# A gated linear-attention kernel: carries over pairs of runs, run ends copied by ScalarE, and the scale's clamp folded into one product

## The reference

```python
mag = np.sqrt(a_re * a_re + a_im * a_im)
scale = np.minimum(mag, 0.999) / (mag + 1e-06)
a_re_n, a_im_n = (a_re * scale, a_im * scale)
for t in range(S):
    ar, ai = (a_re_n[:, :, t, :, None], a_im_n[:, :, t, :, None])
    new_re = ar * S_re - ai * S_im
    new_im = ar * S_im + ai * S_re
    kv = np.einsum('bhd,bhe->bhde', k[:, :, t], v[:, :, t])
    S_re, S_im = (new_re + kv, new_im)
    y[:, :, t] = np.einsum('bhd,bhde->bhe', q[:, :, t], S_re)
...
h = x @ w_in
g = np.maximum(h, 0.0) + np.log1p(np.exp(-np.abs(h)))
x = g @ w_out
...
a = x @ w1
b = x @ w2
h = a * b @ w3
out = h @ w_out2
```

## Time and profile before

| | |
|---|---|
| median of 3 runs | 986.51 us (985.63 to 987.29) |
| profiled execution, its own time | 987.42 us |
| its span in the trace | 985.6 us |
| PE busy | 900.9 us (91%) |
| DVE busy | 608.7 us (62%) |
| ACT busy | 426.5 us (43%) |

### The profile page before, as it was taken

How to read it: one execution, slowest core, us unless ns; L and a number is a source line. 1 busy time by engine, 2 the same in 40 slices (tenths; PEclk the granted TensorE clock), 3 DMA queues, 4 the chain that set the end, 5 groups by cost and what they waited for, 6 DMA issues and landing times.

```text
span 985.6 us, 14230 instructions
## 1 busy us (share of the span) xinstructions
PE 900.9 (91%) x5298; PEld 802.6 (81%) x5298; DVE 608.7 (62%) x982; ACT 426.5 (43%) x612; POOL 70.1 (7%) x56
## 2 busy tenths in 40 slices
PE   0973838999999999999999999999999999999998
PEld 0543738989989989989889999999888888888887
DVE  5978878989988998898999833355221212121211
ACT  4142263575574584674665654588112120202011
POOL 0000000000000000000000000000222222222221
PEclk9995668999999999999999999999999999999999
DMA  9666066174263382480570460320101010101000
GB/s 336 242 192 192 20 178 149 27 213 123 99 167 97 107 191 67 130 207 26 151 199 13 115 143 13 131 105 26 56 0 65 1 65 1 64 0 64 0 33 32
DMA packets 97877, 99.49 MB, mean 101 GB/s; under 512 B 6928, under 2 KB 88848, under 8 KB 97808
## 3 DMA queue, kind: packets, MB, share of 16 engines
q1 hardware_dynamic: 97808, 98.59, 34.8%
HBM read 63.96 MB, written 29.88 MB: 95 GB/s over the span
## 4 chain that ended last, share of the span: by engine, by line
PE 62%; DVE 22%; ACT 6%; DVEq 5%; issue 3%; DMA 1%; ACTq 1%; SPq 0%
PE ps L1318 7%; PE ps L1320 7%; PE ps L1319 7%; PE ps_p L1318 7%; PE ps_p L1320 7%; PE ps_p L1319 7%; PE ps_ay L1354 3%; DVE sp L1196 2%; DVE an L1022 2%; PE ps_ay L1320 2%; PE ps_ay L1319 2%; PE ps_ay L1318 2%; PE ps_k L1320 2%; PE ps_k L1319 2%; PE ps_k L1318 2%
## 5 line engine op out<-in xcount | busy, mean ns | idle before, releaser
L1318 PE MATMUL ps<-g_h,wo_h 128*128 128x384 f32 x384 | 133.3, 347 | 2.0 <-DVE g_l L1203 2.0
L649 POOL TENSOR_TENSOR abl<-ab,abh 128x512 fp32r<-128x512 f32 x48 | 69.2, 1442 | 908.6 <-DVE abh L1301 908.6
L1320 PE MATMUL ps<-g_h,wo_l 128*128 128x384 f32 x384 | 129.6, 338 | 0.0
L1319 PE MATMUL ps<-g_l,wo_h 128*128 128x384 f32 x384 | 129.3, 337 | 0.0
L1318 PE MATMUL ps_p<-x1h,win_h 128*128 128x384 f32 x336 | 116.8, 348 | 6.1 <-DVE sp L1196 6.1
L1320 PE MATMUL ps_p<-x1h,win_l 128*128 128x384 f32 x336 | 112.7, 335 | 0.0
L1319 PE MATMUL ps_p<-x1l,win_h 128*128 128x384 f32 x336 | 112.5, 335 | 0.0
L1354 PE MATMUL ps_ay<-stq,stk 96*128 96x128 f32 x384 | 56.9, 296 | 39.6 <-DVE am L1145 15.4
L1354 PEld LDWEIGHTS ps_ay<-stq,stk 96*128 96x128 f32 x384 | 53.8, 208 | 41.8 <-issue 26.0
L1292 DVE TENSOR_TENSOR ab<-ps_ay,bc 128x512 f32<-128x512 f32 x24 | 16.6, 692 | 114.6 <-ACT bc L918 114.6
L765 ACT ACTIVATE g_h<-sp 128x768 fp32r<-128x768 f32 (+1 forms) x71 | 55.4, 780 | 65.9 <-DVE sp L1196 65.5
(11 more groups left out here) (160 smaller groups left out, 1993.6 us busy)
## 6 DMA issues: line engine op xcount, KB each, us to landing
qk_scr<-tt SPq DMA_DIRECT2D x16, 576.0 KB, 5.1
stq<-qk_scr SPq DMA_DIRECT2D x48, 192.0 KB, 4.8
qk_scr<-pp SPq DMA_DIRECT2D x16, 576.0 KB, 4.0
stk<-qk_scr SPq DMA_DIRECT2D x48, 192.0 KB, 4.5
an<-in_a_re SPq DMA_DIRECT2D x8, 576.0 KB, 3.9
an<-in_a_im SPq DMA_DIRECT2D x8, 576.0 KB, 5.3
qk<-in_q SPq DMA_DIRECT2D x8, 576.0 KB, 7.6
qk<-in_k SPq DMA_DIRECT2D x8, 576.0 KB, 8.9
```

Source lines behind the costliest of these rows:

```text
L649: tensor_tensor(abl[:, m % AR, :], ab[:, m % 2, :], abh[:, m % AR, :].bitcast(F32), ALU.subtract).then_inc(ab_lo, 1)
L1318: mm(o, wh, xh, start=start, stop=False)
L1319: mm(o, wh, xl, start=False, stop=False)
L1320: return mm(o, wl, xh, start=False, stop=stop)
```

## The change

- The carries are computed over pairs of runs: `carry in` multiplies each odd place by the even one before it (72 products of each part), `carry` 1, 2, 4, 8, 16 double over the 24 pair products (w = 24 - s), and `carry out` multiplies the even places by the pair products before them (w = 23). Before there were six doublings over 48 (w = 48 - s).
- The three copies of the run ends move from VectorE to ScalarE (`prep_ends`). VectorE signals `runs_made` behind run 7 and waits for `ends_out` in `ends`.
- `scale start` is gone: the clamp is the first operation of `scale`, as min(r, 1/0.999), and r - 1e6 comes from ScalarE (`prep_root_less`, a copy of 1152 elements with a bias) with the two semaphores `prep_root_made` and `prep_less`.
- Order. In the tables, `ends` and `carry 1` no longer stand ahead of `mask_scores` in step 2: behind it come `ends` and `carry in`, behind the sum `carry` 1 and 2, and 4, 8, 16 and `carry out` in step 3 ahead of its mask. The list `between` in the head changes likewise. In the head, `raw_low(1)` moves between `newton` and `scale`, and `raw_low(3)` from the middle of prep(0)'s carries to behind prep(1)'s `m2`. SP's `load_piece(6)` moves behind `stack_k(0, ...)`. On ScalarE, `prep_root_less(n+3)` stands in step 6 behind `g_high(n, 7)`, ahead of `softplus(n+1, 0)`, and `prep_ends(n+2)` in step 2 behind `k_by_tokens`, between `Abs` and `Exp`.

```diff
-            for i in range(3, 7):
+            for i in range(3, 6):
                 load_piece(i)
...
             for c in range(NCH):
                 stack_k(0, c)
+            load_piece(6)
             load_qk(1)
...
+            def prep_ends(m):
...
+                eng.wait_ge(runs_made, m + 1)
+                for c in range(2):
+                    act(carries[:, c, :, 1:1 + most].rearrange("p g (k r) -> p g k r", r=CR),
+                        ends[:, c, :, 0:NCH - 1, RUN - 1, :], ACT.Copy)
+                act(carries[:, :, :, 1 + most:NR], ends[:, :, :, NCH - 1, RUN - 1, 0:CR - 1], ACT.Copy).then_inc(ends_out, 1)
+
+            def prep_root_less(m):
+                eng.wait_ge(prep_root_made, m + 1)
+                act(te[:, 0, :], te[:, 1, :], ACT.Copy, bias=-1e6).then_inc(prep_less, 1)
...
             raw_high(1)
+            prep_root_less(0)
             raw_high(2)
+            prep_ends(0)
             raw_high(3)
             prep_psquares(0)
             prep_inverse(0)
             prep_squares(1)
             prep_log(1)
             prep_rsqrt(1)
+            prep_root_less(1)
...
                 if i == 1:
+                    prep_ends(1)
                     raw_high(7)
...
             g_high(0, 0, False)
+            prep_root_less(2)
...
                             if att:
                                 k_by_tokens(n + 1, j)
+                            if has_prep and j == 2:
+                                prep_ends(n + 2)
...
                         softplus(n, j + 1, split)
                         g_high(n, j + 1, split)
+                        if nxt_prep:
+                            prep_root_less(n + 3)
...
-            def prep_scale_start(m):
-                ve.tensor_scalar(tr[:, :], te[:, 1, :], 0.999, 1.0, ALU.mult, ALU.min)
-                eng.drain()
...
             def prep_scale(m):
-                ve.scalar_tensor_tensor(out=tr[:, :], in0=te[:, 1, :], scalar=-1e6, in1=tr[:, :],
-                                        op0=ALU.add, op1=ALU.mult)
+                eng.wait_ge(prep_less, m + 1)
+                ve.scalar_tensor_tensor(out=tr[:, :], in0=te[:, 1, :], scalar=1.0 / 0.999, in1=te[:, 0, :],
+                                        op0=ALU.min, op1=ALU.mult)
...
+            def prep_carry_in():
+                t = gp[:, :, :].rearrange("p c (a l) -> p c a l", l=2)
+                n = GC * CR // 2
...
             def prep_carry(s_):
 
-                w = NR - s_
+                w = NPAIR - s_
...
-            before_mask = {0: steps("a", 1), 1: steps("run", 3, 4), 2: steps("run", 7) + ["ends"] + steps("carry", 1),
-                           3: steps("carry", 8, 16, 32), 4: by[3:] + ["p"], 5: []}
-            after_mask = {0: steps("run", 1), 1: steps("run", 5), 2: steps("carry", 2), 3: by[:2], 4: [("q", 0)], 5: ["inverse"]}
-            after_sum = {0: steps("run", 2), 1: steps("run", 6), 2: steps("carry", 4), 3: by[2:3], 4: [("q", 1), "p2"], 5: ["keys"]}
+            before_mask = {0: steps("a", 1), 1: steps("run", 3, 4), 2: steps("run", 7),
+                           3: steps("carry", 4, 8, 16) + ["carry out"], 4: by[3:] + ["p"], 5: []}
+            after_mask = {0: steps("run", 1), 1: steps("run", 5), 2: ["ends", "carry in"], 3: by[:2], 4: [("q", 0)], 5: ["inverse"]}
+            after_sum = {0: steps("run", 2), 1: steps("run", 6), 2: steps("carry", 1, 2), 3: by[2:3], 4: [("q", 1), "p2"], 5: ["keys"]}
...
-            prep(0, True, ["newton", "scale start", "scale"] + steps("a", 0, 1) + steps("run", 1, 2))
+            prep(0, True, ["newton"])
             raw_low(1)
+            prep(0, True, ["scale"] + steps("a", 0, 1) + steps("run", 1, 2))
             prep(0, True, steps("run", 3, 4, 5, 6, 7))
             raw_low(2)
-            prep(0, True, ["ends"] + steps("carry", 1, 2, 4))
+            prep(0, True, ["ends", "carry in"] + steps("carry", 1, 2, 4, 8, 16) + ["carry out"] + by + ["p", ("q", 0), ("q", 1), "p2", "inverse", "keys", "keys end"], first=True)
+            prep(1, False, ["m2"])
             raw_low(3)
-            prep(0, True, steps("carry", 8, 16, 32) + by + ["p", ("q", 0), ("q", 1), "p2", "inverse", "keys", "keys end"], first=True)
-            prep(1, False, ["m2", "newton", "scale start", "scale"] + steps("a", 0, 1))
+            prep(1, False, ["newton", "scale"] + steps("a", 0, 1))
...
-            between = [steps("run", 5), steps("run", 6), steps("run", 7), ["ends"] + steps("carry", 1),
-                       steps("carry", 2, 4), steps("carry", 8, 16), steps("carry", 32) + by[:1], by[1:3], by[3:], [], ["p"], []]
+            between = [steps("run", 5), steps("run", 6), steps("run", 7), [],
+                       ["ends", "carry in"], steps("carry", 1, 2), steps("carry", 4, 8, 16) + ["carry out"] + by[:1],
+                       by[1:3], by[3:], [], ["p"], []]
...
-            prep(2, True, ["newton", "scale start", "scale"] + steps("a", 0))
+            prep(2, True, ["newton"])
             g_low(0, 0, False)
+            prep(2, True, ["scale"] + steps("a", 0))
```

More of the change, by code:

```diff
@@ L31 @@
 CR = CT // RUN
+NPAIR = NR // 2
 GC = G * NCH
@@ L178, in build @@
         prep_rs = sem("prep_rs")
+        prep_root_made = sem("prep_root_made")
+        prep_less = sem("prep_less")
         prep_p = sem("prep_p")
@@ L183, in build @@
         end_ev = sem("end_ev")
+        runs_made = sem("runs_made")
+        ends_out = sem("ends_out")
         te_free = sem("te_free")
@@ L698, in prep_rsqrt @@
                 prep_root_square(m, first)
+            def prep_ends(m):
+                carries = gp[:, :, :].rearrange("p c (g r) -> p c g r", g=G)
+                ends = an[:, :, :].rearrange("p c (g k i r) -> p c g k i r", g=G, i=RUN, r=CR)
+                most = (NCH - 1) * CR
+                eng.wait_ge(runs_made, m + 1)
[6 more added lines that the diff above has]
+                act(te[:, 0, :], te[:, 1, :], ACT.Copy, bias=-1e6).then_inc(prep_less, 1)
             def prep_psquare(m, i):
@@ L941, in _ @@
             carries = gp[:, :, :].rearrange("p c (g r) -> p c g r", g=G)
+            pairs = gp[:, :, :].rearrange("p c (g m l) -> p c g m l", g=G, l=2)[:, :, :, :, 1]
             def cmul(out_r, out_i, a, br, bi, m1, m2):
@@ L948, in cmul @@
                 ve.tensor_tensor(out_r, m1[:, 0], m2[:, 1], ALU.subtract)
-                ve.tensor_tensor(out_i, m1[:, 1], m2[:, 0], ALU.add)
+                last = ve.tensor_tensor(out_i, m1[:, 1], m2[:, 0], ALU.add)
                 eng.drain()
+                return last
             def prep_m2_(m):
@@ L964, in prep_newton @@
                 ve.scalar_tensor_tensor(out=te[:, 1, :], in0=tr[:, :], scalar=1.5, in1=te[:, 1, :],
-                                        op0=ALU.add, op1=ALU.mult)
-                eng.drain()
-            def prep_scale_start(m):
-                ve.tensor_scalar(tr[:, :], te[:, 1, :], 0.999, 1.0, ALU.mult, ALU.min)
+                                        op0=ALU.add, op1=ALU.mult).then_inc(prep_root_made, 1)
                 eng.drain()
             def prep_scale(m):
-                ve.scalar_tensor_tensor(out=tr[:, :], in0=te[:, 1, :], scalar=-1e6, in1=tr[:, :],
-                                        op0=ALU.add, op1=ALU.mult)
+                eng.wait_ge(prep_less, m + 1)
+                ve.scalar_tensor_tensor(out=tr[:, :], in0=te[:, 1, :], scalar=1.0 / 0.999, in1=te[:, 0, :],
+                                        op0=ALU.min, op1=ALU.mult)
                 eng.drain()
             def prep_a(m, c):
-                ve.scalar_tensor_tensor(out=an[:, c, :], in0=an[:, c, :], scalar=-1e-6, in1=tr[:, :], op0=ALU.mult, op1=ALU.mult)
+                ve.scalar_tensor_tensor(out=an[:, c, :], in0=an[:, c, :], scalar=-0.999e-6, in1=tr[:, :], op0=ALU.mult, op1=ALU.mult)
                 eng.drain()
             def prep_run(i):
-                cmul(runs[:, 0, :, i, :], runs[:, 1, :, i, :], runs[:, :, :, i - 1, :],
+                last = cmul(runs[:, 0, :, i, :], runs[:, 1, :, i, :], runs[:, :, :, i - 1, :],
                      runs[:, 0:1, :, i, :].to_broadcast([P, 2, GC, CR]), runs[:, 1:2, :, i, :].to_broadcast([P, 2, GC, CR]),
@@ L987, in prep_run, with prep_carry_start @@
                      ms[:, 2 * GC * CR:4 * GC * CR].rearrange("p (c a r) -> p c a r", c=2, a=GC))
-            def prep_carry_start(even):
+                if i == RUN - 1:
+                    last.then_inc(runs_made, 1)
+            def prep_carry_start(m, even):
                 if even:
@@ L994, in prep_carry_start @@
                     ve.tensor_copy(carries[:, :, :, 0:1], car[:, :, :].unsqueeze(3))
[L995 to L1000, removed]
@@ L1001, in prep_carry_start @@
-                eng.drain()
+                eng.wait_ge(ends_out, m + 1)
+                eng.drain()
+            def prep_carry_in():
+                t = gp[:, :, :].rearrange("p c (a l) -> p c a l", l=2)
+                n = GC * CR // 2
```

(29 more changed lines are left out.)

## The result

The changed kernel takes 995.02 us (994.37 to 995.33, 4 runs) against 986.73 before: ratio 1.0084, 95% interval 1.0068 to 1.0100, slower by 8.3 us. The forecast was 993.8 in a range of 985.5 to 998.0. The profiled execution has a span of 993.4 us (forecast 992.9) and a time of its own of 995.17.

What follows compares the result with a forecast made beforehand. VectorE's chain of waits was taken to bound the head, PE the slots, with VectorE almost without slack. Head -2.5, stretch +7.4 and tile starts +2.4 gave +7.3 us, from 986.5 to 993.8 us; range 985.5 to 998.0.

Steps and rivals of the forecast that it cites:

- The unit: Cost of a complex product on VectorE: 0.60 us fixed plus 0.0032 per element; pairing saves 1.1 us per prep.
- rival D: In the carry products, reading and writing every second element costs double, 2.6 us more per prep: 1014.6 us; chance 0.04.
- The small copies on ScalarE: Three run-end copies between Abs and Exp in step 2: 0.65 us together, bounds 0.4 and 1.2.
- The stretch: Slots, mask 2 to mask 3: VectorE needs 10.77 us against PE's 9.40; 7.4 us lost over six slots.
- One sign: Profile after: PE's stalls for add_relu or the state in steps 4 and 5 rise from 0.3-0.6 to 1.5 us or more.
- The start of a tile: prep_root_less ahead of softplus(n+1, 0) delays down(n, 0) by 0.47 us; five starts, 2.4 us lost.
- The head: Up to 150 us: 4.0 us gained by prep(1)'s newton, less 0.44 and 1.1 lost; net 2.5 us gained.
- Slot 0: Mask 2 to mask 3 there: VectorE 1.37 us late; the start delay before it falls into PE's wait, costing nothing.
- rival E: In the head, weight piece 6 lands late and holds raw_low(6) and mask 0; 3 us late gives 996.8; chance 0.05.
- Rivals A: Head gain alone, neither slot loss arises: 983.2 us, faster; chance 0.15.
- B: In the slots, mask 2 to mask 3 costs nothing, the tile start does: 986.4 us, no change; chance 0.10.
- C: In the slots, mask 2 to mask 3 costs time, the tile start is covered: 991.4 us; chance 0.14.

Runs made afterwards that it cites:

- e1_early: Changed kernel with ScalarE's run-end copies ahead of step 2's Abs, and ends and carry in ahead of mask 2: 986.64 us, ratio 1.0001.
- e7_order_only: Kernel before, with only the slots' tables reordered so that ends and carry 1 stand behind step 2's mask: 997.17 us, ratio 1.0107.
- e3_no_less: Changed kernel with scale start back on VectorE and prep_root_less removed: 992.5 us, ratio 1.0057.
- e6_head: e5_both with, in the head too, ends and carry in ahead of mask 3: 982.51 us, ratio 0.9960.
- e5_both: Changed kernel with the edits of e1_early and e3_no_less together: 983.88 us, ratio 0.9978.

## Why the prediction was right

- **The unit.** Seven products of the worked out lengths: carry 1 takes 1.03 us (105.09 to 106.12 in the head after; 1.03 predicted), the 48-wide one 0.76 (111.29 to 112.05; 0.75 predicted). Reading and writing every second element cost nothing (rival D falls), which is what the Trainium skill, "SBUF — State Buffer", section "Door 1", says of a stride that keeps two accesses in a 16-byte line; the trace agrees.
- **The small copies on ScalarE.** 0.62 us for three, predicted 0.65. The Trainium skill's figure ("VectorE: DVE Perf Modes", section "The TRN2 errata") gives an estimate of 0.27 for one of them, and the trace has 0.27 for the 90-wide one. But they overlap: two take 0.45 together and the third starts 0.35 behind the first, so the three are 0.62 long and not the 0.80 of three in a row.
- **The stretch, 7.4 us lost.** The step that carried the forecast. By the masks' times it is 10.73 to 10.75 us in five of the six slots and 11.07 in slot 2. With the next term, 1.78, 1.51, 1.44 and 1.84 had been worked out for slots 1 to 4, sum 6.6; from `up(n, 1)` to `up(n+1, 1)` they grew by 1.75, 1.80, 1.46 and 1.46, sum 6.5. e1_early takes back 8.3 us by place alone, and e7_order_only loses 10.6 by place alone. One sign was put too high: no stall in steps 4 and 5 of slot 1 is 1.5 us long; there are three, together 1.48, where before there was one of 0.60.
- **The start of a tile, 2.4 us lost.** The size is right: in each of slots 1 to 5 the first product of `down(n, 0)` comes 7.97 to 7.98 us behind `up(n, 1)`, before 7.52 to 7.54, so 0.44 to 0.46 us later where 0.47 was worked out. e3_no_less brings back the 7.52, and its slots 1 to 5 are shorter by 0.83, 0.43, 0.49, 0.45 and 0.13, sum 2.3.
- **The head, 2.5 us gained.** Measured 1.9. The mis-sized step is PE's state product: 0.5 us of waiting was reckoned, and it was 1.50 at the lower clock level (1.77 in e6_head) and 0.75 at the higher one (e1_early). By mask 5 the gain is therefore 1.45 us (118.61 to 117.16) and not 2.4. Another 0.44 come between mask 5 and the first scores of tile 1, where no term stood: that stretch ends with the load of `vt` and is 32.23 us before, 31.79 after, and 30.82 in e7_order_only, whose head is that of the kernel before. So the 1.9 is in part luck.
- **Slot 0, 1.4 us lost.** Measured 0.5. PE reaches its higher clock level 4.5 us after the first scores of tile 1, in the kernel before 6.6 us after them (0.93 granted from 150 to 175 us, 0.85 before). That fits the missing 0.9, and was not tried by itself.
- **Piece 6** landed 6.9 us after its issue at 72.2, and `raw_low(6)` was not held: rival E falls. Rivals A, B and C each needed at least one of the two slot terms to be zero, and neither was.

The sum by the trace: head -1.9, slot 0 +0.5, slots 1 to 4 +6.5, slot 5 +1.7, together 6.8 of the span's 7.8 us. The last 1.0 lies behind 650 us, where the kernels execute the same instructions: the stretch to the first moe2 split is 0.3 longer (so it is in e1_early), and the rest takes 300.55 us against 299.8 to 300.0 in the nine other kernels. I put that down to the execution; it was not tried by itself. So the terms that carried the forecast hold one by one, but that the span came within 0.5 us of it (993.4 against 992.9) is partly luck: the head gained 0.6 less and slot 0 lost 0.9 less than worked out, and the last 1.0 was in no term.

## What to carry to other kernels

Where one engine paces and another follows with no slack, list the follower's fixed points, the instructions that must wait for the pacing engine, and sum the follower's work between two of them: work moved from in front of such a point to behind it is paid as soon as that sum is above the pacing engine's own time between the two points, whatever the total did. Handing a small operation to another engine costs that engine's queue at that place; look at what is queued behind it (here `Exp`, `Ln` and a whole softplus) and put it where that engine waits anyway. A saving of work is worth something only in a stretch in which the follower is late.

## What the runs showed of the hardware

TensorE's clock in the head moved without any change on TensorE. While the small products of tile 0 run, the eight products of 0.88 us at the higher level come first at 106.51 in the kernel before, at 109.07 in the changed one, although its products start 3.55 us earlier, and in e6_head not at all: its window from 100 to 125 us has a granted clock of 0.50 (2.4 GHz is 1.00). e1_early has the changed kernel's head, instruction for instruction, and has them at 103.31. So the moment of the rise differs by 5.8 us between executions of one order of work, and VectorE's wait for the state product of step 2 with it, 0.75 or 1.50 us. What decides it stays open.

Single executions of one kernel differ by more. Ten of e3_no_less run from 986.58 to 994.54 us, eleven of e5_both from 977.93 to 985.98, and in both the fastest, about 5 us ahead of the next, has by far the highest granted clock over the whole span (0.972, the others 0.959 to 0.967). Neither of these two executions has a trace, so where they gain the time can't be read. Whoever compares two single executions can take such a difference for the effect of an edit.
